# Scores and state products on 64-row tiles, scores ahead of the value products, and one compact state in two buffers

## What is computed

```python
for t in range(S):
    kt, vt, qt = (k[:, :, t], v[:, :, t], q[:, :, t])
    m_new = np.maximum(f_gate[:, :, t] + m, i_gate[:, :, t])
    f_stab = np.exp(f_gate[:, :, t] + m - m_new)
    i_stab = np.exp(i_gate[:, :, t] - m_new)
    C = f_stab * C + i_stab * einsum('bhd,bhe->bhde', vt, kt)
    n = f_stab * n + i_stab * kt
    h_tilde = einsum('bhde,bhe->bhd', C, qt)
    denom = max(abs(n . qt), 1.0)
    y[:, :, t] = sigmoid(o_gate[:, :, t]) * h_tilde / denom
```

## Time and profile before

| | |
|---|---|
| median of 3 runs | 288.86 us (288.39 to 289.34) |
| profiled execution | 291.4 us, of which the span of its instructions is 289.3 us |
| TensorE busy | 264.7 us, 91% |
| VectorE busy | 180.0 us, 62% |
| ScalarE busy | 115.4 us, 40% |
| GpSimd busy | 85.7 us, 30% |
| data moved | 25.68 MB, mean 89 GB/s |

### The profile page before, as it was taken

The page is one execution under the profiler, slowest core; times in us unless marked ns, Lnnn a source line. Parts: engine busy times, 40 slices in busy tenths (PEclk is TensorE's granted clock), DMA queues, the critical chain, the costliest instruction groups (busy, mean ns, idle before and its releaser), DMA issues.

```text
span 289.3 us, 5204 instructions
## 1 busy us (share of the span) xinstructions
PE 264.7 (91%) x1964; PEld 247.3 (85%) x1964; DVE 180.0 (62%) x401; ACT 115.4 (40%) x212; POOL 85.7 (30%) x102
## 2 busy tenths in 40 slices
PE   0598788999999999999999999999999999999675
PEld 0587677679799999999999997899999999999564
DVE  7988877486878568535866303537653168742991
ACT  2664545488444432443432223322232332232731
POOL 4415578903654553155004000000040000130710
PEclk9999999999999999999999999999999999999988
DMA  7699987664765143220000010000000100000101
GB/s 219 155 274 321 302 265 219 212 198 124 208 189 132 57 142 91 84 68 3 0 0 2 3 66 2 0 0 2 0 2 23 45 1 2 0 2 0 56 13 68
DMA packets 26289, 25.68 MB, mean 89 GB/s; under 512 B 13977, under 2 KB 22009, under 8 KB 26265
## 3 DMA queue, kind: packets, MB, share of 16 engines
q1 hardware_dynamic: 21976, 18.72, 22.2%
q10 hardware_dynamic: 4288, 6.64, 7.1%
HBM read 23.34 MB, written 2.02 MB: 88 GB/s over the span
## 4 chain that ended last, share of the span: by engine, by line
PE 74%; DVE 7%; issue 7%; POOL 5%; ACT 4%; DMA 1%; SPq 0%; ACTq 0%; POOLq 0%; DVEq 0%
PE shared L1172 30%; PE h_ps L1306 22%; PE s_ps L1210 4%; PE hv_ps L1191 2%; PE s_ps L1244 2%; PE hv_ps L1195 2%; DVE gate L1039 2%; PE shared L1271 2%; PE h_ps L1244 2%; POOL qs L597 2%; PE shared L1221 1%; DMA mask_sb<-mask 1%; PE shared L1318 1%; DVE prob L930 1%; PE shared L1256 1%
## 5 line engine op out<-in xcount | busy, mean ns | idle before, releaser
L1104 DVE SCALAR_TENSOR_TENSOR h_lo<-shared,h_hi 128x384 fp32r<-128x384 f32 x48 | 26.5, 557 | 40.2 <-ACT h_hi L824 40.1
L1306 PE MATMUL h_ps<-ch_hi,h_hi 128*128 128x320 f32 x144 | 45.4, 315 | 0.0
L1306 PE MATMUL h_ps<-ch_hi,h_lo 128*128 128x320 f32 x144 | 44.5, 309 | 0.0
L824 ACT ACTIVATE h_hi<-shared 128x384 fp32r<-128x384 f32 x48 | 23.1, 488 | 53.2 <-PE shared L1172 50.1
L1306 PE MATMUL h_ps<-ch_lo,h_hi 128*128 128x320 f32 x144 | 44.3, 308 | 0.0
L1172 PE MATMUL shared<-u_hi,ch_hi 128*128 128x384 f32 x96 | 33.1, 344 | 0.1
L1172 PE MATMUL shared<-u_lo,ch_hi 128*128 128x384 f32 x96 | 32.6, 339 | 0.0
L1172 PE MATMUL shared<-u_hi,ch_lo 128*128 128x384 f32 x96 | 32.5, 339 | 0.0
L1210 PE MATMUL s_ps<-q_in,k_in 128*128 128x128 f32 x192 | 27.1, 300 | 3.9 <-DMA q_in<-qT 3.9
L1210 PEld LDWEIGHTS s_ps<-q_in,k_in 128*128 128x128 f32 x192 | 25.2, 211 | 6.1 <-DMA q_in<-qT 4.5
L1039 DVE SCALAR_TENSOR_TENSOR gate<-x,conv_sb,gate 128x384 f32<-128x384 f32 x44 | 29.0, 668 | 1.0
(11 more groups left out here) (181 smaller groups left out, 550.3 us busy)
## 6 DMA issues: line engine op xcount, KB each, us to landing
G_all<-G_scratch SPq DMA_DIRECT2D x11, 512.0 KB, 5.8
o_sig<-on ACTq DMA_DIRECT2D x2, 960.0 KB, 6.7
k_in<-kT SPq DMA_DIRECT2D x24, 80.0 KB
q_in<-qT SPq DMA_DIRECT2D x24, 80.0 KB
kn_in<-kn SPq DMA_DIRECT2D x12, 160.0 KB, 4.3
v_in<-vn SPq DMA_DIRECT2D x12, 160.0 KB, 4.8
stage<-ch ACTq DMA_DIRECT2D x3, 640.0 KB, 4.3
out<-o_sb SPq DMA_DIRECT2D x12, 160.0 KB, 1.8
```

The costliest lines, as they stand in the source:

```text
L824: act.activation(h_hi[i % 3][:], ps_of(key)[:, 0:T], ACT.Relu).then_inc(hi_ready, 1)
L1104: took(dve.scalar_tensor_tensor(out=h_lo[i % 3][:], in0=ps_of(key)[:, 0:T], scalar=0.0, in1=h_hi[i % 3][:].bitcast(F32), op0=ALU.max, op1= ...
L1306: last = pe.matmul(h2_ps[t][:, 0:DM], a[:, tile_cols(t)], w[:, f, :], start=(f == 0 and n == 0), stop=(f == FT - 1 and n == 2))
```

## The change

- `k_in` becomes two buffers of [128, 512] without padding; keys of group g lie on the partitions of group g alone. A score product reads 40 rows at partition 0 or 64 (`r = slice(64*g, 64*g + D)`) of both operands. Heads of the two groups alternate.
- Both k buffers serve both batches; keys of unit u wait for the scores of unit u-2.
- `apart` is gone. `state` has two buffers and is written once by VectorE for each unit. State products read 40 rows and write columns 0 to 40 or 64 to 104, so that they take the two diagonal corners of the array.
- In TensorE's order the state products of unit u-1 come first, then the scores of unit u, then the value products of unit u-1. `hv_ps` is opened once for a whole unit (first product) and closed with the last head.
- `delta` alternates the two groups instead of doing four heads of one and then four of the other.
- The score wait on `prob_ready` is one for both groups; VectorE waits for both groups' scores before the first `prob` product.
- The memsets of `k_in` and `apart` are gone, and the first keys are loaded before the wait for them. The last unit's `kn_in` load of each batch, which nobody reads, is left out.

```diff
-        k_in = [sb("k_in0", [P, 2, HG * L]), sb("k_in1", [P, 2, HG * L], at=a_at + 4 * S)]
+        k_in = [sb(f"k_in{k}", [P, HG * L]) for k in range(2)]
...
-        state = sb("state", [ROWS, HG * D1])
-        apart = [sb(f"apart{k}", [P, 2, HG * D1]) for k in range(2)]
+        state = [sb(f"state{k}", [ROWS, HG * D1]) for k in range(2)]
...
             def k_chunk(u):
-                users = k_users(u)
-                if len(users) > 1:
-
-                    sp.wait_ge(s_ready, 2 * (users[-2] + 1))
+                if u >= 2:
+
+                    sp.wait_ge(s_ready, 2 * (u - 1))
...
-            sp.wait_ge(zeroed, 4)
             k_chunk(0)
+            sp.wait_ge(zeroed, 2)
             q_chunk(0)
...
-            dve.memset(k_in[0][:], 0.0).then_inc(zeroed, 1)
...
             def attention(b, n):
                 u = b * NC + n
                 if n < NC:
+                    dve.wait_ge(s_ready, 2 * u + 2)
                     for g in range(2):
                         w = 2 * u + g
                         dve.wait_ge(exp_ready, w + 1)
-                        dve.wait_ge(s_ready, w + 1)
...
-                    new = apart[(u + 1) % 2]
-                    grown(new[0:64, 0, :], slice(0, 64))
-                    last = grown(new[64:ROWS, 1, :], slice(64, ROWS)).then_inc(apart_ready, 1)
-                    if n < NC - 2:
-                        last = grown(state[:], slice(0, ROWS))
-                        took(last, key)
...
+                    took(grown(state[(u + 1) % 2][:], slice(0, ROWS)), key)
...
+                v = u - 1
+                if n >= 1 and v >= 1:
+                    pe.wait_ge(ht_ready, v)
+                if n >= 2:
+
+                    pe.wait_ge(qs_ready, with_state(v))
+                    done(pe, ("delta", v - 1))
+                    for j in range(HG):
+                        for g in range(2):
+                            r = slice(64 * g, 64 * g + D)
+                            pe.matmul(hv_ps[64 * g:64 * g + D1, tile_cols(j)], state[v % 2][r, j * D1:(j + 1) * D1],
+                                      qs[v % 2][r, tile_cols(j)], start=(j == 0), stop=False)
+                if n < NC:
+
+                    pe.wait_ge(q_loaded[k], 32 * (u // 2 + 1))
+                    pe.wait_ge(k_loaded[k], 32 * (u // 2 + 1))
+                    if u >= 1:
+                        pe.wait_ge(prob_ready, 2 * u)
+                    for j in range(HG):
+                        for g in range(2):
+                            r = slice(64 * g, 64 * g + D)
+                            last = pe.matmul(s_ps[g][:, tile_cols(j)], k_in[k][r, tile_cols(j)],
+                                             q_in[k][r, tile_cols(j)], start=True, stop=True)
+                            if j == HG - 1:
+                                last.then_inc(s_ready, 1)
                 if n >= 1:
 
-                    v = u - 1
                     pe.wait_ge(prob_ready, 2 * v + 2)
                     pe.wait_ge(v_loaded[v % 3], 16 * (v // 3 + 1))
...
                     for j in range(HG):
...
                         for g in range(2):
                             last = pe.matmul(hv_ps[64 * g:64 * g + D1, tile_cols(j)], v_in[v % 3][:, g * HG + j, :],
-                                             prob[(2 * v + g) % 4][:, tile_cols(j)], start=(n < 2), stop=True)
+                                             prob[(2 * v + g) % 4][:, tile_cols(j)],
+                                             start=(n < 2 and j == 0), stop=(j == HG - 1))
                     last.then_inc(hv_ready, 1)
```

More of the change, by code:

```diff
@@ L357, in y_waits, with kn_users @@
                 eng.wait_ge(y_ready, y_made(v))
[L359 to L365, removed]
+        def kn_users(u):
+            return [x for x in range(u % 2, u + 1, 2) if x % NC < NC - 1]
         def used_h(eng, n):
@@ L449, in kn_chunk @@
                 t0 = (u % NC) * L
-                if u >= 2:
-                    full(sp, ("delta", u - 2 if (u - 2) % NC < NC - 1 else u - 3))
+                users = kn_users(u)
+                if len(users) > 1:
+                    full(sp, ("delta", users[-2]))
                 sp.dma_start(kn_in[u % 2][:], kn[u // NC, t0:t0 + L, :]).then_inc(kn_loaded[u % 2], 16)
@@ L1178, in attention @@
                 if n >= 1:
-                    v = u - 1
                     pe.wait_ge(prob_ready, 2 * v + 2)
                     pe.wait_ge(v_loaded[v % 3], 16 * (v // 3 + 1))
[L1183 to L1187, removed]
-                    for j in range(HG):
[L1189 to L1192, removed]
-                                          start=True, stop=False)
+                    for j in range(HG):
@@ L1200, in attention @@
                     token_hidden(0, n - 4)
-                if n < NC:
-                    pe.wait_ge(q_loaded[k], 32 * (u // 2 + 1))
-                    pe.wait_ge(k_loaded[k_buffer(u)], 32 * len(k_users(u)))
-                    for g in range(2):
-                        w = 2 * u + g
-                        if w >= 2:
-                            pe.wait_ge(prob_ready, w - 1)
-                        for j in range(HG):
-                            last = pe.matmul(s_ps[g][:, tile_cols(j)], k_in[k_buffer(u)][:, g, tile_cols(j)],
-                                             q_in[k][:, tile_cols(j)], start=True, stop=True)
-                        last.then_inc(s_ready, 1)
                 if n < NC - 1:
@@ L1216, in attention @@
                     pe.wait_ge(wv_ready, with_next(u))
-                    pe.wait_ge(kn_loaded[k], 16 * (u // 2 + 1))
-                    for h in range(H):
-                        g, j = divmod(h, HG)
-                        m = 64 if g == 0 else D
-                        last = pe.matmul(ps[64 * g:64 * g + m, j * D1:(j + 1) * D1],
-                                         kn_in[k][:, h * D:h * D + m], wv[:, h, :], start=True, stop=True)
+                    pe.wait_ge(kn_loaded[k], 16 * len(kn_users(u)))
+                    for j in range(HG):
+                        for g in range(2):
+                            h = g * HG + j
+                            m = 64 if g == 0 else D
+                            last = pe.matmul(ps[64 * g:64 * g + m, j * D1:(j + 1) * D1],
+                                             kn_in[k][:, h * D:h * D + m], wv[:, h, :], start=True, stop=True)
                     last.then_inc(shared_full, 1)
```

17 lines of the change are left out of this document (4 added, 13 removed).

## The result

The change makes the kernel slower. Its median is 294.17 us (292.17 to 294.88, 4 runs) against 288.62 (288.04 to 289.34, 4 runs) for the kernel before in the same measurement: a ratio of 1.018, 95% interval 1.0123 to 1.0236. Forecast were 285.8 us and a range up to 289.2. The profiled execution took 294.88 us, its span is 292.0. Medians here are over all runs of a kernel, while the ratios leave out runs well above its own best; where a kernel scatters and the two disagree, I go by the median.

What follows compares the result with a forecast made beforehand. Batch 0 was taken as bound by transfers until about 41.1 us, batch 1's attention mostly by TensorE. Terms 0 - 0.7 - 0.5 - 1.98 - 0.11 + 0.15 = -3.1 us off the 288.86 median gave 285.8 us, range 282.8 to 289.2.

Steps and rivals of the forecast that it cites:

- Scores: Score matmuls on 64-row tiles run side by side on TensorE: -0.89 us for each unit.
- State products: State matmuls as diagonal corners of the array still take 8 rounds: 0 gained.
- Rivals 2 and 3: Row tiles take turns: 290.0 us, chance 0.08; the state's two corners take turns: up to 291.9 us, chance 0.08.
- `delta`: Alternating groups in `delta`'s 16 matmuls overlaps the column halves: -0.1 us (0 to -0.25).
- Order: `turn_y` waits for `ht` in batch 1: +0.33 us for each step n = 2 to 4, +0.78 in n = 5.
- Steps n = 2 to 4: Batch 1 steps, saving on scores and `delta` less the wait for `ht`: -1.98 us together.
- n = 5: Batch 1 step without `delta`: -0.89 for scores, +0.78 for the wait for `ht`, -0.11 us.
- n = 6: Last step of batch 1, where state and values now differ in shape: +0.15 us.
- n = 0 and 1: First steps of batch 1, where only VectorE's two state copies shorten the chain: -0.5 us.
- Batch 0's tail: From `qs` at 43.79 us, TensorE through the last values earlier: -0.7 us (-0.3 to -1.2).
- rival 4: TensorE's clock rises a step later or falls again in batch 0: +3 us, so 288.8 us, chance 0.12.
- Rival 1: Batch 0's transfers follow TensorE's buffer releases, so units 1 to 4 gain too: about 282.8 us, chance 0.10.

Runs made afterwards that it cites:

- e7: The changed kernel with GpSimd's wait (e1), but scores behind the value products as before the change: 289.11 us, ratio 0.9926 to before.
- e6: The kernel before (128-row operands, single key buffer) with only the new TensorE order of state, scores, values: 293.94 us, ratio 1.02.
- e4: The changed kernel plus four unused filler products ahead of the scores in batch 0's steps: 293.08 us, ratio 1.0179 to before.
- e5: e1 plus the four unused filler products in batch 0's steps: 288.39 us, ratio 0.9994 to before.
- e8: The changed kernel with filler, batch 1's exponents and exps behind the next hidden tile's copy, `kept` and `qs` after them: 288.64 us, ratio 0.9995.
- e9: e8 with the scores behind the value products, as in the kernel before: 287.23 us, ratio 0.9933 to before.
- e1: The changed kernel with GpSimd's weighing of batch 1's values, from unit 7, waiting for that unit's exponents: 289.09 us, ratio 1.0014 to before.
- e3: The kernel before with unit 7's values loaded ahead of its keys: 293.57 us, ratio 1.0152 to before.
- before again: The kernel before, unchanged, run for a second profile: 288.8 us, span 287.0 us.
- e10: e9 without the four filler products: 289.73 us, ratio 1.0004 to before.
- e2: The changed kernel with keys of units 7 to 11 loaded only after the previous unit's scores, as with one buffer: 290.35 us, ratio 0.9979.

## Why the prediction was wrong, point by point

- *Scores* (0.89 us forecast): measured 2.05 - 1.16 = 0.89. *State products* (0): measured, no turns. Rivals 2 and 3 are out. Rival 3's rule (the Trainium skill, TensorEngine Tiling (Array Packing), "Gotcha 1: PSUM Pressure") isn't borne out for these tiles, which write different partitions of the bank: 16 in 1.07 us. *`delta`* (-0.1): 0.61 to 0.66 instead of 0.76, right.
- *Order* (+0.33 and +0.78): 0.35 and 0.79, right for batch 1. Without the wait (`e7`) a step is 0.24 us shorter. For batch 0 I had no term for the order; on padded tiles (`e6`) 1.8 us are lost there, on the new tiles with filler some 0.6 (`e4`, `e5`, `e8` against `e9`), which is within the scatter.
- *Steps n = 2 to 4* (-1.98): -1.98, right. *n = 5* (-0.11): +0.22, the sign wrong by a size under half a us. In `e7` this step takes 9.08 us against 9.68 before, so the tiles gave 0.60 there where I had 0.89; why is open. *n = 6* (+0.15): right.
- **The step that failed:** "The single key buffer of batch 1 costs nothing today ... With two, unit 7's and 8's loads come earlier and may delay weight pieces ... I take 0." I asked what the earlier loads would delay in the queue and not which engine they would release. They released GpSimd into the eight exponents of VectorE that the earlier trace rows shows on the chain. For n = 0 and 1 I took -0.5 us, and the exponents did start 14.6 us behind the token block instead of 15.3; but the stretch from the token block to `delta` 7 grew by 82.50 - 58.67 = 23.8 us against 20.45 in both executions of before, +3.4, and 1.2 more by the low clock behind it. `e1` and `e3` show it from both sides, at 4 to 5 us in the time.
- *Batch 0's tail* (-0.7): +2.1 here against before again, which is rival 4. With the clock up the term isn't shown either way: the three kernels with filler start their token blocks on average at 56.3 us, the four with the tiles of before at 56.65. I had given it +3 us at a chance of 0.12; its own size in the kernel after is less certain: `e4` has the token block 1.7 us earlier, and its median is 1.1 us lower, yet its ratio, 1.0179, is no better than the change's 1.018. In `e9` against `e10` it is worth (1.0004 - 0.9933) x 289 = 2.1 us, or 2.5 by the medians.
- *Rival 1:* its sign seemed to be there (`wv` of unit 4 at 39.08 instead of 41.16), but `e1` and `e2`, with the same batch 0, have it at 41.2 and 41.1, and the unchanged kernel had it at 40.4 the second time. It is scatter, and nothing here shows that the landings follow TensorE.
- *A rival was missing:* the collision at unit 7, on the slower side. The sum of the parts: -3.1 forecast; +3.9 for unit 7 (3.4 + 0.5), +1.2 for the clock behind it, +2.8 for the tail (2.1 + 0.7) and +0.3 for n = 5 make +5.1, and the spans are 292.0 - 287.0 = 5.0 us apart (medians: 5.55).
- *What stays open.* With the collision mended (`e1`), and batch 0's clock too (`e5`, `e8`), the profiled spans are 1.2, 1.1 and 2.0 us under before's 287.0, while the medians are level with it (289.09, 288.39 and 288.64). These profiled executions are the lowest of ten in `e1` and `e8` and the second lowest in `e5`, so they flatter the kernels, and a single profile doesn't show what the other executions lose. That the low clock around each idle stretch comes and goes between executions would do it (`e9` had it at 76.0 to 82.8 with 2.52 us of idle time, `e8` shows none with 2.36), but I have only argued that. Why TensorE loses time in batch 0 of `e6` with its clock up is open as well.

## What to carry to other kernels

When a buffer is added, ask which engine the earlier landing will start, and what runs on its neighbour at that moment: a wait for a DMA can be what keeps two engines apart, and the single added wait of `e1` was worth nearly all that the change had cost. Cheaper matmuls in a stage that waits for transfers bought nothing here, and came with a low clock that reached into the stage behind it. Where a stage is tuned this closely, take a second profile of the kernel before ahead of any sum: two executions here differ by 2.3 us in the span, more than any term of my sum.

## What the hardware showed that I had not expected

- Matmuls of 40 rows by 41 columns on the two diagonal corners of the array, into different partitions of one PSUM bank, run beside each other: the two of a pair start 0.007 us apart, and it comes to 0.053 us each for 128 columns at full clock. The row pairs of the scores, 40 by 128 into two banks, take 1.16 us for 16, where one 128-row tile after the other takes 2.05.
- Several GpSimd instructions in a row can hold off one VectorE instruction all the way: two exponents from 76.29 to 80.29 us. The timeline of the kernel after, narrowed to them:

```profile
76.29 4.00 DVE L919 SCALAR_TENSOR_TENSOR prob<-G_all,A_col,mask_sb 128x128 f32<-128x128 f32 x2
```

  GpSimd pays almost nothing for it (`wv` 0.78 instead of 0.74 us, `kept` 0.51 instead of 0.46); VectorE pays nearly all.
- An exponent with its mask in PSUM took at most 0.350 us in all fourteen profiles, one with both inputs in SBUF up to 3.274 (`e6`).
- The same products on fewer rows, in a stage bound by transfers, came with a clock that rose late or fell again: it was up for good only from 32.4 to 45.0 us in the five kernels without filler (the kernel after had it up at 31.24 and at half from 38.07 to 44.9), against 21.4 to 25.1 in the four with filler and 21.2 to 23.1 in the five with padded products. The kernel before can fall again too, only sooner: its second execution had the full clock from 12.8 to 16.2 us and then half until 23.0.
